# Second-layer tail of a fused DFT and two-MLP kernel: other buffers, banks and order for the last ten units; first units and output copies placed anew

## The reference

```python
X = np.fft.fft(np.fft.fft(x, axis=1), axis=2).real        # (2, 3008, 256)

h = X @ w_in                                              # first layer, 256 -> 2048
r = np.maximum(h, 0.0)
x1 = (r * r) @ w_out                                      # 2048 -> 256

h = x1 @ w_in2                                            # second layer
P = a[0] + a[1] * h + a[2] * h * h + a[3] * h * h * h
Q = 1.0 + abs(b[0]) * abs(h) + abs(b[1]) * h * h
out = (P / (Q + 1e-06)) @ w_out2
```

## Time and profile before

| | |
|---|---|
| median of 3 runs | 1067.92 us (1065.12 to 1068.27) |
| profiled execution | 1066.06 us |
| its span in the trace | 1064.3 us |
| mean granted clock of PE | 0.99 of full |

### The profile page before, as it was taken

One profiled execution on the slowest core, in us unless ns is written; L12 is line 12 of the kernel. 1 busy time (PEld: TensorE's weight loads), 2 busy tenths in 40 slices (PEclk: granted clock), 3 DMA queues, 4 the chain that ended last, 5 costly groups with the idle time before them and its releaser, 6 DMA issues.

```text
span 1064.3 us, 13867 instructions
## 1 busy us (share of the span) xinstructions
PE 1024.4 (96%) x5288; PEld 869.6 (82%) x5288; DVE 882.4 (83%) x836; ACT 889.0 (84%) x928; POOL 567.7 (53%) x302
## 2 busy tenths in 40 slices
PE   9999899999999999999999999999999999999776
PEld 8798778888888888888888888888888888888665
DVE  2466798988888888988988988988988888888877
ACT  2358899999998998998998999989989988888574
POOL 0227666556566565565565565565655655555332
PEclk9999999999999999999999999999999999999888
DMA  9764000001001001001001001001001001000000
GB/s 251 274 213 179 1 1 21 1 1 40 1 1 40 1 1 40 1 1 40 2 1 40 1 1 40 1 1 40 1 1 40 1 1 36 1 21 1 0 20 15
DMA packets 22580, 36.50 MB, mean 34 GB/s; under 512 B 1601, under 2 KB 17394, under 8 KB 21874
## 3 DMA queue, kind: packets, MB, share of 16 engines
q1 hardware_dynamic: 22514, 35.63, 10.3%
HBM read 23.78 MB, written 11.81 MB: 33 GB/s over the span
## 4 chain that ended last, share of the span: by engine, by line
PE 79%; ACT 8%; DVE 6%; issue 5%; POOL 1%; DMA 0%; DVEq 0%; ACTq 0%; SPq 0%; POOLq 0%
PE ps L738 41%; PE ps L729 20%; PE ps L764 7%; PE ps L753 5%; PE ps L681 3%; DVE den_s L600 2%; ACT g_value L481 2%; PE ps L701 2%; ACT seed_s L496 1%; PE ps L690 1%; ACT g_value L460 1%; ACT seed_s L499 1%; ACT out_s L512 1%; DVE g_value L601 1%; ACT minus_s L454 1%
## 5 line engine op out<-in xcount | busy, mean ns | idle before, releaser
L738 PE MATMUL ps<-g_hi,w_out_lo 128*128 128x512 f32 (+1 forms) x764 | 302.1, 395 | 26.5 <-POOL g_lo L418 17.3
L416 POOL CAST g_hi<-g_value 128x1024 fp32r<-128x1024 f32 (+1 forms) x94 | 96.8, 1030 | 397.6 <-DVE g_value L618 397.6
L738 PE MATMUL ps<-g_hi,w_out_hi 128*128 128x512 f32 (+1 forms) x764 | 300.8, 394 | 0.0
L738 PE MATMUL ps<-g_lo,w_out_hi 128*128 128x512 f32 (+1 forms) x764 | 299.0, 391 | 0.0
L418 POOL TENSOR_TENSOR g_lo<-g_value,g_hi 128x1024 fp32r<-128x1024 f32 (+1 forms) x94 | 223.8, 2381 | 7.5
L408 POOL TENSOR_TENSOR g_lo<-g_value,g_hi 128x1024 fp32r<-128x1024 f32 (+1 forms) x86 | 203.8, 2370 | 2.6 <-ACT g_hi L469 2.6
L738 PEld LDWEIGHTS ps<-g_hi,w_out_lo 128*128 128x128 f32 x764 | 145.5, 190 | 58.6 <-POOL g_lo L418 19.3
L600 DVE SCALAR_TENSOR_TENSOR den_s<-den_s,b_abs,ps 128x1024 f32<-128x1024 f32 x88 | 112.7, 1281 | 73.3 <-ACT g_value L481 73.2
L738 PEld LDWEIGHTS ps<-g_hi,w_out_hi 128*128 128x128 f32 x764 | 145.6, 191 | 29.4
L738 PEld LDWEIGHTS ps<-g_lo,w_out_hi 128*128 128x128 f32 x764 | 146.4, 192 | 25.7
L609 DVE SCALAR_TENSOR_TENSOR den_s<-den_s,seed_s 128x1024 f32<-128x1024 f32 x88 | 113.3, 1288 | 25.7 <-ACT seed_s L499 25.7
(11 more groups left out here) (79 smaller groups left out, 1792.9 us busy)
## 6 DMA issues: line engine op xcount, KB each, us to landing
x_s<-x SPq DMA_DIRECT2D x16, 384.0 KB, 7.6
out_t<-out_s SPq DMA_DIRECT2D x11, 512.0 KB, 3.0
w_out_unsplit_lo<-w_out SPq DMA_DIRECT2D x2, 2048.0 KB, 18.6
tw_s<-twiddle SPq DMA_DIRECT2D x1, 3012.0 KB, 18.6
y_hi_dram<-y_stage_hi SPq DMA_DIRECT2D x10, 256.0 KB, 3.1
y_lo_dram<-y_stage_lo SPq DMA_DIRECT2D x10, 256.0 KB, 3.3
y_hi<-y_hi_dram SPq DMA_DIRECT2D x10, 256.0 KB, 2.8
y_lo<-y_lo_dram SPq DMA_DIRECT2D x10, 256.0 KB, 3.1
```

The source lines that it names most:

```text
L738: last = nc.tensor.matmul(acc[:, mb, 0:n], w[a][:, f, mb * P:(mb + 1) * P], g[c][:, i, 0:n], start=(f == 0 and j == 0), stop=(f == FB - 1 ...
```

## The change

Once up1 of unit 95 is done, the weights of the first layer's up product are dead, and after down1 of unit 95 those of its down product. The change uses their memory for the tail: num and the low part get eight blocks (`num_of`, `lo2_of`), den and the seed four each (`den_of`, `seed_of`). h2 rotates over three pairs of banks (0-1, 2-3, 4-5) from unit 86 on. The tail's order is written anew on PE, ACT, DVE: down1(95) comes right after up2(86); DVE keeps z's low part ahead of the reads; ACT runs two units ahead with the absolute value and the cubic. Unit 95 is divided and split by halves: ACT copies both high parts, POOL and DVE make one low part each, and PE takes the first half of the unit through both output blocks and then the second.

In the first units, tile 0's z goes to banks 6 and 7, h2 of unit 1 too, and PE's waits change accordingly; the DFT's banks swap their order (`UV_BANKS`) so that these are free. The output copy of a tile moves on ACT from behind Square to behind the high-part copy of the step before.

Cut to its core:

```diff
 COLUMNS = (K1 - 1) * BATCH * N2 + BATCH * LAST_K2
-UV_BANKS = (2, 3, 6, 7)
...
 DRAIN = STEPS - SKEW
+H2_FREE = 3
+WIDE_BUFS = 4
 EARLY = TILES - 2
 CLOSING = STEPS - 2
+AHEAD = 2
...
+            flat = w.rearrange("p k f -> p (k f)")
+            return flat[:, n * 2 * TN:(n + 1) * 2 * TN].rearrange("p (i n) -> p i n", i=2)
+
+        def lo2_of(m):
+
+            if m < DRAIN:
+                return g2_lo_s[:, m % NUM_BUFS, :, 0:width(m)]
+            n = (m - DRAIN) % (2 * WIDE_BUFS)
+            return free_block(w_in1_s[n // WIDE_BUFS], n % WIDE_BUFS)[:, :, 0:width(m)]
+
+        def num_of(m):
+
+            if m < DRAIN:
+                return num_s[:, m % NUM_BUFS, :, 0:width(m)]
...
         def den_of(m):
 
-            return r_s[:, m % R_BUFS, :, 0:width(m)] if m >= LAST else den_s[:, m % 2, :, 0:width(m)]
+            if m < LAST:
+                return den_s[:, m % 2, :, 0:width(m)]
+            return free_block(w_out1_raw, m % WIDE_BUFS)[:, :, 0:width(m)]
 
         def seed_of(m):
 
-            return den_s[:, m % 2, :, 0:width(m)] if m >= LAST else seed_s[:, :, 0:width(m)]
+            if m <= DRAIN:
+                return seed_s[:, :, 0:width(m)]
+            return free_block(w_out1_free, m % WIDE_BUFS)[:, :, 0:width(m)]
 
         def h2_banks(m):
 
-            return ps[:, 0:2, :] if m >= DRAIN and m % 2 == 0 else h2_p
+            if m == 1:
+                return o_p
+            if m < DRAIN:
+                return h2_p
+            at = 2 * ((m - DRAIN) % H2_FREE)
+            return ps[:, at:at + 2, :]
+
+        def z_banks(t):
+
+            return o_p if t == 0 else z_p
...
                 act.wait_ge(h2_ready, m + 1)
                 if m >= LAST:
                     act.wait_ge(prod1_done, STEPS)
-                after(act, g2_done, m - 2 if m >= LAST + R_BUFS else m - 1 if m < LAST else 0)
+                    after(act, g2_done, m + 1 - WIDE_BUFS if m >= LAST + WIDE_BUFS else 0)
+                else:
+                    after(act, g2_done, m - 1)
                 nc.scalar.activation(den_of(m), h2_banks(m)[:, :, 0:width(m)], ACT.Abs, scale=b1).then_inc(v_done, 1)
 
             def cubic_h2(m):
-                n = width(m)
-                after(act, prod2_done, m + 1 - NUM_BUFS)
-                nc.scalar.activation(num_s[:, m % NUM_BUFS, :, 0:n], h2_banks(m)[:, :, 0:n], ACT.Identity, bias=a2, scale=a3
+                if m >= DRAIN:
+                    act.wait_ge(plus_ready, STEPS)
+                    after(act, prod2_done, m + 1 - 2 * WIDE_BUFS if m >= DRAIN + 2 * WIDE_BUFS else 0)
+                else:
+                    after(act, prod2_done, m + 1 - NUM_BUFS)
+                nc.scalar.activation(num_of(m), h2_banks(m)[:, :, 0:width(m)], ACT.Identity, bias=a2, scale=a3
...
-                if m >= LAST:
-                    act.wait_ge(g2_done, m - 1)
+                if m > DRAIN:
+                    act.wait_ge(prod1_done, STEPS)
+                    after(act, rec_done, m + 1 - WIDE_BUFS if m > DRAIN + WIDE_BUFS else 0)
...
+            def keep_z_hi(t):
+                n = 2 * pairs(t)
+                act.wait_ge(prod1_done, (t + 1) * UNITS)
+                after(act, h2_ready, t * UNITS)
...
-                if down is not None and down % UNITS == UNITS - 1:
-                    keep_out(down // UNITS)
...
-                if second == DRAIN:
-                    abs_h2(DRAIN + 1)
-                if first is not None and first >= HEAD:
-                    keep_hi1(first)
+                    keep_z_hi(summed // UNITS)
+                if second is not None:
+                    from_h2(second)
+                if s >= HEAD:
+                    keep_hi1(s)
+                if multiplied is not None and multiplied % UNITS == UNITS - 1:
+                    keep_out(multiplied // UNITS)
                 if second is not None:
...
+            from_h2(DRAIN)
+            keep_z_hi(TILES - 1)
+            from_h2(DRAIN + 1)
+            from_q(DRAIN)
+            from_q(DRAIN + 1)
+            for m in range(LAST, LAST + AHEAD):
+                from_h2(m)
+            for m in range(LAST, STEPS):
+                from_q(m)
+                if m == LAST + 1:
+                    keep_out(TILES - 2)
+                if unit(m + AHEAD) is not None:
+                    from_h2(m + AHEAD)
+            keep_hi2(hi2_of(CLOSING), num_of(CLOSING), CLOSING + 1, CLOSING - 1)
+            for i in range(2):
+                keep_hi2(hi2_of(STEPS - 1)[:, i, :], num_of(STEPS - 1)[:, i, :], STEPS + i, STEPS - 2)
+            keep_out(TILES - 1)
...
+            def divide(m, half=None):
+                part = slice(None) if half is None else half
+                count = m + 1 if half is None else m + 1 + half
+                den, seed, num = (v[:, part, :] for v in (den_of(m), seed_of(m), num_of(m)))
...
-                if before is not None and s <= STEPS:
+                if before is not None:
                     divide(before)
-                if summed is not None and summed % UNITS == UNITS - 1 and s < STEPS:
+                if summed is not None and summed % UNITS == UNITS - 1:
                     keep_z_lo(summed // UNITS)
                 if second is not None:
                     read_h2(second)
-                if summed == STEPS - 1:
-                    keep_z_lo(TILES - 1)
-                if before is not None and s > STEPS:
-                    divide(before)
-            reciprocal(STEPS - 1)
-            keep_lo2(STEPS - 2)
-            quotient(STEPS - 1)
-            keep_lo2(STEPS - 1)
+
+            divide(DRAIN - 1)
+            keep_z_lo(TILES - 1)
+            read_h2(DRAIN)
+            read_h2(DRAIN + 1)
+            divide(DRAIN)
+            divide(DRAIN + 1)
+            read_h2(LAST)
+            for m in range(LAST + 1, STEPS):
+                read_h2(m)
+                divide(m - 1)
+            m = STEPS - 1
+            divide(m, 0)
+            keep_lo2(lo2_of(CLOSING), num_of(CLOSING), hi2_of(CLOSING), 1)
+            divide(m, 1)
+            keep_lo2(lo2_of(m)[:, 1, :], num_of(m)[:, 1, :], hi2_of(m)[:, 1, :], 3)
...
-                else:
-                    after(pe, h2_read, m - 1 if m > DRAIN else m)
+                elif m == 2:
+                    pe.wait_ge(h2_read, 1)
+                elif m > 2 and m != LAST:
+                    pe.wait_ge(h2_read, m - 2 if m > LAST else m - 1 if m == DRAIN + 1 else m)
...
-                if m % UNITS == 0:
-                    after(pe, z_lo, m // UNITS)
+                if m % UNITS == 0 and m >= 2 * UNITS:
+                    pe.wait_ge(z_lo, m // UNITS)
...
-                if m % UNITS == 0:
-                    after(pe, out_kept, m // UNITS)
+                if m == 0:
+                    pe.wait_ge(h2_read, 2)
+                elif m % UNITS == 0:
+                    pe.wait_ge(out_kept, m // UNITS)
...
+            def down2_by_halves(m):
+                g, n = (hi2_of(m), lo2_of(m)), width(m)
+                for i in range(2):
+                    if i == 0:
+                        pe.wait_ge(g2_lo, CLOSING + 1)
+                    else:
+                        pe.wait_ge(dve_lo2, 2)
+                    f = 2 * (m % UNITS) + i
+                    for mb, done in enumerate((half_done, prod2_done)):
                         for j, (a, c) in enumerate(((1, 0), (0, 1), (0, 0))):
-                            last = nc.tensor.matmul(o_p[:, mb, 0:width(m)], w_out2_s[a][:, f, mb * P:(mb + 1) * P],
-                                                    g[c][:, i, 0:width(m)], start=False, stop=(f == FB - 1 and j == 2))
-                    last.then_inc(done, 1)
+                            last = nc.tensor.matmul(o_p[:, mb, 0:n], w_out2_s[a][:, f, mb * P:(mb + 1) * P],
+                                                    g[c][:, i, :], start=False, stop=(f == FB - 1 and j == 2))
+                        if i == 1:
+                            last.then_inc(done, 1)
...
-                if s == STEPS:
-                    down1(STEPS - 1)
-                if s == STEPS + 1:
-                    up2(following)
+
+            down1(STEPS - 2)
+            up2(DRAIN)
+            down1(STEPS - 1)
+            up2(DRAIN + 1)
+            down2(DRAIN - 2)
+            up2(LAST)
+            down2(DRAIN - 1)
+            up2(LAST + 1)
+            for m in range(LAST + 2, STEPS):
+                up2(m)
+                down2(m - 4)
+            for m in range(STEPS - 4, STEPS - 1):
+                down2(m)
+            down2_by_halves(STEPS - 1)
```

127 lines of the change are left out of this document (53 added, 74 removed).

## The result

| | before | after |
|---|---|---|
| median (runs) | 1068.06 us (4: 1065.12 to 1068.27) | 1050.95 us (4: 1050.03 to 1051.58) |
| profiled execution | 1066.06 us | 1051.58 us |
| its span | 1064.3 us | 1049.8 us |

The ratio is 0.9845, with a 95% interval of 0.9826 to 0.9865: faster by 1.55%. The forecast was 1049.3 with a range of 1044.5 to 1056. The profiled execution is 14.5 us shorter where 16.8 were forecast; the medians are 17.1 apart. That the second lies so near the forecast is in part luck: the execution the sum started from was 2.0 us under its median, and the one profiled after lies 0.6 above its own.

The account below looks back on a forecast made before the run. It took PE, busy 96% of the span, as the bound of the dense part and DVE as the tail's. Copies 8.8, first units 1.9, entry with tail 5.9, end 0.2: 1066.06 - 16.8 = 1049.3 us, range 1044.5 to 1056.

Parts of the forecast that it names:

- Output copies: Tile boundaries: PE no longer waits for the previous tile's output copy; nine stops of 0.86 us and one of 1.1, 8.8.
- First units: Tile 0's new banks remove PE stops; up2 of unit 3 starts at 144.2 instead of 146.10, 1.9 us (ends 0 and 4.6).
- Front: Start of the kernel with the warm-up matmuls, code unchanged: forecast 0 us.
- Entry: Start of the last ten units: z_hi follows up2 of unit 87, at 982.9 instead of 988.76; with DVE idle, 5.1 us earlier.
- Tail: DVE from z_lo to the end of unit 94's division: 59.5 us without stops plus 3.2 for meeting POOL, 62.7.
- The rival without a collision: In the tail POOL finds its turns without holding DVE, so the 3.2 us term goes: 1046.1 us, chance 0.17.
- the stops at L481: DVE's four tail waits for ACT's cubic, 10.4 us, put down to value buffers; if order caused them, 1059.7 us.
- End: From unit 94's division to the last copy's end: 9.4 us instead of 9.6; 7.7 at full clock, 11.8 at half.
- Part is given back: Rival: ACT late at tile boundaries and a tail stall behind tile 10's copy lose 6.4 us: 1055.7 us, chance 0.24.
- Half clock for the whole tail: Rival: PE, idling in every tail unit, stays at half clock and the kernel gets slower: 1071.8 us, chance 0.04.
- z_lo some 16 us earlier: Sign of a right forecast: DVE's low part of the last tile's z comes near 973 us.
- the last copy near 1044: Sign of a right forecast at the kernel's end: the last output copy comes near 1044 us.

Follow-up runs that it names:

- the second profile of the change: The changed kernel run once more as it is, nothing altered: median 1050.52 us, its profiled execution 1049.26 us.
- the other profile of the old tail: The changed kernel with buffers, banks and order of the last ten units put back as before: 1055.68 us.
- the extra matmuls: The changed kernel plus 14 unused 392-column matmuls ahead of each down2 of units 92, 93 and 94: 1048.79 us.
- the alternating order: The changed kernel with DVE putting a read between every two divisions from unit 87 on: 1049.42 us.
- both fillings: On the changed kernel with the alternating order: 42 unused matmuls at the end and 7 zero-multiplying ones ahead of up2 of unit 3; 1047.10 us.

## Why the prediction was right, and where it was off

- *Output copies (8.8, measured 9.1 in the profile; taking them back gave 9.1 in the stretch that holds them and 8.0 between medians).* Right, the mechanism and the full price: ten waits gone, the tile period 79.65 us (forecast 79.7), no push of ACT that reaches PE.
- *First units (1.9, measured 0.1).* The chain was right to the tenth: up2 of unit 3 starts 1.9 us earlier once the late front is taken off. What failed is the step from there to the sum: the prediction took the earlier start as the gain and put the clock behind PE's new stop at nothing, without a reason; in the profile it fell, 0.66 from 145 to 150 us, and took 1.8 back (1.6 by the clock alone). Where it doesn't fall (the second profile of the change), the 1.9 stays, and the kernel before can have such a fall as well, as the run with the old first units shows. A difference of two single profiles measured here which of the two had it.
- *Front (0, measured -1.0).* Not a part of the change. The warm-up took 5.22 to 6.69 us over the profiles, at unchanged code, and the first up1 began between 66.6 and 68.4 us, which shifts a single execution by as much as a small term. A sum made against one profiled execution has this error on each side.
- *Entry (5.1, measured 4.7).* DVE waited 2.49 us for z_hi, as forecast ("some 3").
- *Tail (62.7, measured 62.1).* DVE has no gap, and the meeting is where I put it, on L678 and L682 of unit 87. Its price was 2.7 instead of 3.2: I took nearly all of POOL's 3.4, but by the four rows the two engines' operations overlap more at their ends. The rival without a collision falls. That the stops at L481 came from buffers was right too: they came back with three value buffers and nothing else undone, 9.2 us of them. Against the other profile of the old tail the term is nothing instead of 1.4, so the 0.9 is met within what one profile can tell.
- *End (9.4, measured 9.5).* Right, half clock included. At full clock it is 8.5, not the 7.7 of the low end: the prediction had the second half's split ready before PE is through unit 94, but at full clock it is not, and PE stops for it, since POOL holds DVE up by 0.8 us.
- *Rivals.* "Part is given back" falls in its place: the copies kept their full gain, and though PE waited 6.4 us ahead of down2 of unit 86 and ran at 0.68 there, ACT waited only 0.26 us for the copy of tile 10 and DVE did not stop. The time lies between this rival and the forecast; what was given back in the profile came from the clock at 145 us and the front. "Half clock for the whole tail" falls: 1.00 from 1000 to 1030 us although PE waits 1.2 to 1.3 us in each unit. The Trainium skill (TensorE: Matmul & The Clock Gate, Part 1) calls the throttled state the default that activity lifts; the extra matmuls agree (0.60 and 0.87 without, 1.00 with them), but the waits of one unit did not bring that state back from 1000 to 1030 us; the clock was low where the waits were of 6.4, 3.4 and 2.6 us.
- *"z_lo some 16 us earlier" and "the last copy near 1044"* were off by 3 us each (975.84, 1046.88), by the front, the first units and the entry. The sum itself gives 1044.6 for the copy.

The shortest median is that of the change with the alternating order and both fillings, 1047.10 us; without the filling at 145 us it is 1047.47 beside it, which can't be told apart.

## What to carry over

When a chain of three engines stops in turn, look for the one resource that ties the last to the first (here a value buffer that down2 had to free): with it undone alone, the new order and the other buffers won nothing that shows. Give the engine of the chain its operations in an order in which a split on POOL meets a read from PSUM and not another division. And where PE waits a microsecond or two, price the stop with and without a fall of the clock behind it; a few matmuls of no use in the wait, over before it ends, can keep the clock up.

## What the runs showed that I had not expected

- A stop of 1.9 us at 145 us was followed by half clock in four of nine profiles, of one and the same kernel in one of two. Cost: 1.6 us each. A like stop at 137.71 us had it as well.
- The warm-up of 8 matmuls took between 5.22 and 6.69 us from one execution to the next.
- 42 extra matmuls made the kernel faster (1048.79 against 1050.52); they ran in PE's idle time, with up to 1.0 us left of each wait.
- POOL's last subtraction meets DVE at the end as well: 1.39 us for an operation of 0.56, and at full clock PE stops for it.
